# First MLP step taken row by row: centring, rounding and the order of TensorE's first products

## The reference

```python
# 1. retention: q, k, v (2, 8, 768, 64), blocks of 64 with decay lam per head -> x (2, 768, 512)
# 2. mixing:
X = np.fft.fft(x, axis=1)            # along the sequence
X = np.fft.fft(X, axis=2)            # along the features
u = x + np.real(X)
mu = np.mean(u, axis=-1, keepdims=True)
var = np.mean((u - mu) ** 2, axis=-1, keepdims=True)
un = (u - mu) / np.sqrt(var + 1e-06)
x = u + np.maximum(un @ w_ch1, 0.0) @ w_ch2          # w_ch1 (512, 2048), w_ch2 (2048, 512)
# 3. gate: five-tap causal convolution over the sequence, sigmoid, times (x @ w_val), times w_out
```

## Time and profile before

| | |
|---|---|
| time, median of 3 runs | 427.54 us (427.39 to 428.16) |
| the profiled execution's own time | 427.97 us |
| its span in the trace | 426.3 us |
| TensorE busy | 418.8 us, 98% of the span |
| VectorE, ScalarE, GpSimd busy | 281.3, 187.0 and 211.4 us |
| granted TensorE clock, mean | 1.00 |

### The profile page before, as it was taken

The page is one execution under the profiler, slowest core; times in us unless marked ns, Lnnn a source line. Parts: engine busy times, 40 slices in busy tenths (PEclk is TensorE's granted clock), DMA queues, the critical chain, the costliest instruction groups (busy, mean ns, idle before and its releaser), DMA issues.

```text
span 426.3 us, 6828 instructions
## 1 busy us (share of the span) xinstructions
PE 418.8 (98%) x2626; PEld 353.6 (83%) x2626; DVE 281.3 (66%) x451; ACT 187.0 (44%) x354; POOL 211.4 (50%) x139
## 2 busy tenths in 40 slices
PE   8999999999999999989999999999999999999997
PEld 8788888788888888879898988888788888888886
DVE  5658989759345579948667652617998859669400
ACT  2355842584213457474644432254254342624212
POOL 3543431443876396857787793445645338300000
PEclk9999999999999999999999999999999999999999
DMA  7997801430420231232232323321321321002022
GB/s 235 352 330 228 255 3 33 144 120 8 143 98 24 78 100 49 92 106 99 100 100 98 101 98 110 119 81 64 121 68 37 100 93 49 0 2 99 0 100 98
DMA packets 14863, 44.09 MB, mean 103 GB/s; under 512 B 1904, under 2 KB 2160, under 8 KB 14832
## 3 DMA queue, kind: packets, MB, share of 16 engines
q1 hardware_dynamic: 14832, 43.67, 30.9%
HBM read 40.52 MB, written 3.15 MB: 102 GB/s over the span
## 4 chain that ended last, share of the span: by engine, by line
PE 81%; DVE 12%; ACT 2%; DMA 2%; issue 2%; SPq 1%; DVEq 0%; ACTq 0%
PE ps L732 8%; PE ps L734 8%; PE ps L733 8%; PE ps L661 6%; PE ps L669 6%; PE ps L662 6%; PE ps L568 3%; PE ps L840 3%; PE ps L839 3%; PE ps L838 3%; PE ps L816 3%; PE ps L530 3%; PE ps L817 3%; PE ps L818 3%; PE ps L676 3%; PE ps L675 3%
## 5 line engine op out<-in xcount | busy, mean ns | idle before, releaser
L984 ACT ACTIVATE hh<-ps 128x512 fp32r<-128x512 f32 x32 | 18.9, 603 | 88.3 <-PE ps L669 88.3
L1358 DVE SCALAR_TENSOR_TENSOR hl<-ps,hh 128x512 fp32r<-128x512 f32 x32 | 21.6, 688 | 49.2 <-ACT hh L984 49.2
L1442 DVE SCALAR_TENSOR_TENSOR xT<-u_pad,cw,xT 128x768 f32<-128x768 f32 (+2 forms) x48 | 52.6, 1164 | 0.0
L1595 POOL TENSOR_TENSOR w2l_b<-raw_b,w2h_b 128x1024 fp32r<-128x1024 f32 x12 | 30.7, 2557 | 32.3 <-ACT w2h_b L947 32.3
L1595 POOL TENSOR_TENSOR w2l_a<-raw_a,w2h_a 128x1024 fp32r<-128x1024 f32 x12 | 31.1, 2592 | 29.9 <-ACT w2h_a L947 26.4
L732 PE MATMUL ps<-hh,w2h_a 128*128 128x512 f32 x96 | 37.9, 395 | 1.6 <-DVE xT L1374 1.6
L732 PE MATMUL ps<-hh,w2h_b 128*128 128x512 f32 x96 | 38.1, 397 | 0.1
L734 PE MATMUL ps<-hh,w2l_b 128*128 128x512 f32 x96 | 37.9, 395 | 0.0
L733 PE MATMUL ps<-hl,w2h_b 128*128 128x512 f32 x96 | 37.9, 395 | 0.0
L734 PE MATMUL ps<-hh,w2l_a 128*128 128x512 f32 x96 | 37.5, 391 | 0.0
L733 PE MATMUL ps<-hl,w2h_a 128*128 128x512 f32 x96 | 37.5, 390 | 0.0
(11 more groups left out here) (252 smaller groups left out, 1193.0 us busy)
## 6 DMA issues: line engine op xcount, KB each, us to landing
raw_a<-in_mlp SPq DMA_DIRECT2D x25, 512.0 KB, 3.6
raw_b<-in_mlp SPq DMA_DIRECT2D x23, 512.0 KB, 3.6
chunks<-in_qkv SPq DMA_DIRECT2D x12, 512.0 KB, 6.4
chunks<-in_qkv SPq DMA_DIRECT2D x22, 256.0 KB, 5.7
out<-out_sb SPq DMA_DIRECT2D x11, 256.0 KB, 2.0
raw_a<-in_val SPq DMA_DIRECT2D x2, 512.0 KB, 3.7
raw_b<-in_out SPq DMA_DIRECT2D x2, 512.0 KB, 5.5
seq_c<-const_seq SPq DMA_DIRECT2D x1, 768.0 KB, 7.9
```

The costliest lines, as they stand in the source:

```text
L984: nc.scalar.activation(hh[:, slot, j], ps[j][:, :], ACT.Relu).then_inc(s_hh, 1)
L1358: stt(hl[:, slot, j], ps[j][:, :], 0.0, hh[:, slot, j].bitcast(F32), ALU.max, ALU.subtract).then_inc(s_hl, 1)
L1442: stt(xT[:, b, r, tok], u_pad[b][:, r, PAD - d + tok.start:PAD - d + tok.stop], cw[:, K - 1 - d, r:r + 1], xT[:, b, r, tok], ALU.mult, ALU ...
L1595: tt(lo, raw_, hi.bitcast(F32), ALU.subtract).then_inc(s_w2l, 1)
```

## The change

On ScalarE and VectorE the first piece goes row by row: `centre(0)` is four instructions of one row, each counting `s_cen`, and `cen_hi(0)` four copies, each waiting for its own row. The counts that others wait for follow (`centred(i)` is the count at which piece i is centred). VectorE's `centre(1)` stands ahead of `radix4(N - 1)` and of step 0's low part. On TensorE step 0 has a function of its own, `first_hidden()`: the products of the high parts of the tokens for both banks come first, then those of the low parts for both. Behind it, and ahead of step 1's first layer, stand now `hid_transform(N - 2)` and `hid_transform(N - 1)`, the transforms 10 and 11.

```diff
         def high_parts(i):
-            return 2 * (i + 1) - (i >= 2)
+            return centred(i) - (i >= 2)
+
+        def centred(i):
+            return R + 2 * i
...
-                if n == NC + 4:
-                    pe.wait_ge(s_cen, 4)
+                if n >= NC + 4:
+                    pe.wait_ge(s_cen, centred(n - NC - 4))
...
             def mlp_hidden(st):
-                if st.m == 0:
-                    pe.wait_ge(s_pr, 2 * N)
...
+            def first_hidden():
+                pe.wait_ge(s_pr, 2 * N)
+                pe.wait_ge(s_w1h, 1)
+                pe.wait_ge(s_w1l, 1)
+                for j in range(2):
+                    cols = slice(j * P, (j + 1) * P)
+                    for r in range(R):
+                        if j == 0:
+                            pe.wait_ge(s_cenh, r + 1)
+                        mm(ps[j][:, :], w1h_a[:, r, cols], cen_h0[:, r], start=r == 0, stop=False)
+                        mm(ps[j][:, :], w1l_a[:, r, cols], cen_h0[:, r], start=False, stop=False)
+                for j in range(2):
+                    cols = slice(j * P, (j + 1) * P)
+                    for r in range(R):
+                        if j == 0 and r % 2 == 0:
+                            pe.wait_ge((s_cenl[0], s_cenl[1])[r // 2], r // 2 + 1)
+                        m = mm(ps[j][:, :], w1h_a[:, r, cols], cen_l0[:, r], start=False, stop=r == R - 1)
+                    m.then_inc(s_h, 1)
...
-            mlp_hidden(steps[0])
+            first_hidden()
+            hid_transform(N - 2)
+            hid_transform(N - 1)
...
                 if after:
                     mlp_hidden(after)
-                if st.m == 0:
-                    hid_transform(N - 2)
-                    hid_transform(N - 1)
...
             def cen_hi(i):
+                if i == 0:
+                    for r in range(R):
+                        act.wait_ge(s_cen, r + 1)
+                        copy(of_block(cen_h, i)[:, r], of_batch(acc_of, i)[:, r]).then_inc(s_cenh, 1)
+                    return
...
                 mu = wide(i)
+                if i == 0:
+
+                    for r in range(R):
+                        tt(of_batch(acc_of, i)[:, r], of_batch(u, i)[:, r], mu, ALU.subtract).then_inc(s_cen, 1)
+                    return
...
             centre(0)
             cen_lo(0)
+            centre(1)
             radix4(N - 1)
             hidden_lo(steps[0])
-            centre(1)
```

More of the change, by code:

```diff
@@ L638, in variance @@
                 pe.wait_ge(s_vl, b + 1)
-                pe.wait_ge(s_cen, 2 * len(pieces))
+                pe.wait_ge(s_cen, centred(len(pieces) - 1))
                 if b:
@@ L950, in squares @@
                 b = pieces[i].b
-                act.wait_ge(s_cen, 2 * (i + 1))
+                act.wait_ge(s_cen, centred(i))
                 act.wait_ge(s_mean, 2 * (b + 1))
@@ L971, in cen_hi @@
                     pair = slice(2 * e, 2 * e + 2)
-                    act.wait_ge(s_cen, 2 * i + e + 1)
+                    act.wait_ge(s_cen, centred(i) + e - 1)
                     if i == 2 and e == 0:
@@ L1277, in cen_lo @@
             def cen_lo(i):
-                dve.wait_ge(s_cenh, high_parts(i) - 1)
+                dve.wait_ge(s_cenh, high_parts(i) - 1 if i else 2)
                 tt(of_block(cen_l, i)[:, 0:2], of_batch(acc_of, i)[:, 0:2], of_block(cen_h, i)[:, 0:2].bitcast(F32),
@@ L1282, in cen_lo @@
                 if i == 0:
-                    dve.wait_ge(s_cenh, 2)
+                    dve.wait_ge(s_cenh, R)
                     tt(of_block(cen_l, i)[:, 2:4], of_batch(acc_of, i)[:, 2:4], of_block(cen_h, i)[:, 2:4].bitcast(F32),
@@ L1291, in combine_tokens @@
                 (b11, b21), (b12, b22) = ([of_batch(acc_of, i)[:, 2 * d:2 * d + 2] for d in range(2)] for i in (1, 2))
-                dve.wait_ge(s_cen, 6)
+                dve.wait_ge(s_cen, centred(2))
                 dve.wait_ge(s_f, 4 * R)
```

## The result

| | before | after |
|---|---|---|
| median, 6 runs each | 427.55 us (427.39 to 428.16) | 429.28 us (428.62 to 429.47) |
| profiled execution | 427.97 | 429.47 |
| its span | 426.3 | 427.7 |

The ratio of the times is 1.0034, 95% interval 1.0022 to 1.0047, or +1.45 us (0.94 to 2.0). It is estimated from all the runs; the two medians by themselves lie 1.73 us apart. Measured again beside the kernel before, with more runs, the ratio was 1.0021 (1.0009 to 1.0034), +0.9 us. The forecast was +0.92.

The account below looks back on a forecast made before the run. TensorE, busy 98% of the span, was taken to bound the kernel. A gain of 0.83 us from rows and a loss of 1.75 from the moved transforms gave +0.92, so 428.5 us, range 427.7 to 429.1 (8 in 10).

Parts of the forecast that it names:

- What bounds the kernel: Whole span: TensorE busy 98%; time won or lost between step 0's first layer and the MLP's middle goes on.
- Rows one by one: Start of step 0's first layer: row-wise centring and rounding gain 0.83 us, bounds 0.56 and 1.22.
- High parts first: Step 0's product order: changes nothing; low parts ready by 79.6, wanted at about 80.1, otherwise a microsecond late.
- the gain of the rows "alone": Start of step 0, forecast for the kernel with the transforms back: about 0.75 us gained, ratio 0.998.
- The moved transforms: Transform 10 behind step 0: TensorE waits 1.51 us for spectrum copies plus 0.24 restart, loss 1.75 us.
- The sum: Whole kernel: -0.83 + 1.75 = +0.92 us, giving 428.5 us, slower by 0.21%.
- The wait on the copies: Rival at transform 10: copies are ready, wait does not bind, only the gain stays, 426.7 us; chance 0.05.
- second late wait: Rival in the second batch, at 107.57 or from 147 to 191: 0.5 to 1.5 us more; chance 0.08.
- The clock: Rival after the new 1.5 us wait: TensorE's clock falls, 2.3 us for 10 products, 430.8 us; chance 0.02.

Follow-up runs that it names:

- old order: Kernel with the copies first, but step 0's products per bank, high parts then low parts; first mean to step 1's second layer 28.30 us, ratio 1.0001.
- transforms back: Changed kernel with transforms 10 and 11 back behind step 1's first layer; first mean to step 1's second layer 28.38 us, ratio 0.9999.
- only the transforms moved: Kernel before with only transforms 10 and 11 moved behind step 0's first layer and centre(1) ahead of chunk 11's fold; ratio 1.0035.
- copies first: Changed kernel with ScalarE's spectrum copies of transforms 8 and 9 ahead of step 0's two relus; 427.13 us, ratio 0.9970.
- the change again: Changed kernel without edit, timed again beside the kernel before; ratio 1.0021, first mean to step 1's second layer 29.30 us.
- Copies first, pairs: Kernel with the copies first, but piece 0 centred and rounded in pairs of rows as before; ratio 0.9999.

## Why the prediction was right, step by step

**What bounds the kernel.** Held. From step 1's second layer to the end the traces of before and of the change take 324.32 and 324.22 us, and the eight others lie between these, so what happened at 77 to 92 us went unchanged to the end. The wait near 191 moved along (191.48 to 192.95) and stayed 1.6, as I had read from VectorE's idle time at 146.69.

**Rows one by one.** Forecast 0.83, measured 0.75 or 0.76. The chain of waits of the changed kernel, to be held against the earlier trace rows:

```profile
76.93 0.25 PE ps L684
...
79.15 0.23 PE ps L684
...
80.99 1.85 PE ps L691 x8
...
84.32 0.71 PE ps L592 x4
...
92.68 0.23 PE ps L754
```

Transform 9 ends at 76.93 instead of 76.42, so 0.51 us are to be taken off each time of this trace. The four rows then started at 76.20, 76.74, 77.31 and 77.90; I had 76.26, 76.72, 77.30 and 77.89. Step 0 ended at 80.99 + 1.85 - 0.51 = 82.33, I had 82.26. Most of the 0.07 between these lies behind the rows: the last 16 products took 3.69 us (79.15 to 82.84), and I had 3.64. VectorE's four rows took 2.48 us, that is 0.60 apart at 0.68 each; I had 0.59. The prediction also gave a rule of the Trainium skill ("VectorE: DVE Perf Modes", "The DRAIN you can't avoid") by which each row would start only after the one before it had emptied the pipe, 0.68 apart, 2.72 for the four. I had read that section too narrowly: it says as well that a next operation that is not held starts earlier. The trace agrees with that sentence, and not with the rule taken alone.

**High parts first, at nothing.** The reason that I gave held (the low parts would have come late, and did in "old order"), and its price in the change is nothing. The size was off: I had the second pair a microsecond late, because I took it to be wanted together with the first, at 78.5; it is wanted two products later, and in "old order" it started 0.58 late. Nor were the low parts wanted at 78.5 in the kernel before, as I wrote, but at 79.25. And I named only half of what the order does. It frees bank 0 late, and I did not say what covers that: the moved transforms. That this term came out right is luck, since the cover happened to be part of the change; the gain of the rows "alone" that I put on record for the kernel with the transforms back was wrong for this reason, by 0.8 us.

**The moved transforms.** Forecast a loss of 1.75; measured 1.75 by itself ("only the transforms moved") and 1.80 in the change (29.32 against 27.52 with the copies first). In the change TensorE's wait ended at 83.81, with the 0.51 taken off, and I had 83.77. The first four products afterwards took 0.71 us in the chain instead of 0.44, 0.27 more for the restart where I had put 0.24.

**The sum.** +0.92 forecast, +1.00 and +0.98 measured in the stretch (in the chain, 92.68 - 0.51 against 91.16: 1.01). The time moved by 1.45 in the first comparison and by 0.9 in the second. In the traces of before and of the change what goes beyond the 1.00 is the 0.50 at the start, and "the change again" showed that the start varies by itself. That the same is behind the 1.45 of all runs is likely and not shown. My range reached to +1.6 for the spread of medians, and the spread was needed: +1.45 lies within it, but not within the +1.3 that the terms gave, and the median itself, 429.28, stands 0.2 above the 429.1 that I had named as the upper end. The size of the change's own effect in the traces needed none of it.

**The rivals.** The wait on the copies did bind. No second late wait came: VectorE ended the second batch's fold 5.1 us before TensorE wanted it, where I had counted on 4.8 and part of it lost:

```profile
103.27 0.69 DVE L1251 SCALAR_TENSOR_TENSOR yy<-sd,yy 128x514 f32<-128x514 f32 x1
...
109.07 0.38 PE L616 MATMUL ps<-seq_c,yy 128*128 128x128 f32 x2
```

The clock did not fall behind the new wait; the windows of the change (length, busy time of TensorE, its weight loads, VectorE, ScalarE and GpSimd, granted clock, DMA share, GB/s) show 1.00, the 2.4 GHz level, in it and behind it:

```profile
82.00:84.30 2.30, 0.82 (x4) 0.35 (x2) 1.63 (x4) 1.98 (x9) 1.97 (x1) 1.00 0.00 0
84.30:88.00 3.70, 3.68 (x21) 3.29 (x22) 0.00 (x0) 3.70 (x8) 0.53 (x2) 1.00 0.46 146
```

## What to carry to other kernels

Work that is moved to fill a gap takes its waits along. Look up what the thing waited for is queued behind on its own engine: here five copies stood behind a relu that needed the very last product, so the filling could not start until the gap was over, and moving one line behind two others on ScalarE turned +1.0 us into -0.8. Second, an edit that brings a result forward pays only if the next thing wanted is also early and the buffer it leaves is free in time; try the parts in pairs before calling one of them useless. Third, compare stretches between two fixed instructions in the traces. The one here repeated within 0.02 us in the two traces of the same kernel, where the first mean alone scattered by 0.9 over the ten traces.

## What was not expected of the hardware

The start of an execution varies more than all the rest. The first mean, at about 73.7 us, stood anywhere between 73.39 and 74.26 in ten traces, while what follows step 1's second layer took 324.22 to 324.32 in all ten. A late start of chunk 0's first product (5.19 to 5.77) did not go with a late mean in every trace: 5.48 went with 73.39, and 5.29 with 74.26. These two show where the scatter lies. "Transforms back", chunk 3's first product and the first mean:

```profile
17.31 1.16 PE L534 MATMUL ps<-chunks 64*128 64x128 f32 x16 [0.43 <-DMA chunks<-in_qkv]
...
74.26 1.45 PE L636 MATMUL ps<-out_sb,ones 128*128 128x512 f32 x4
```

"Copies first, pairs":

```profile
16.45 1.16 PE L534 MATMUL ps<-chunks 64*128 64x128 f32 x16
...
73.39 1.45 PE L636 MATMUL ps<-out_sb,ones 128*128 128x512 f32 x4
```

From chunk 3's first product to the first mean both take 56.95 or 56.94 us, and all ten traces lie between 56.94 and 56.96. So the whole scatter arises in the first 17 us. There TensorE waits in every trace at least once for a load of `in_qkv`, for 0.2 to 1.1 us at a time and at a different chunk from trace to trace. That these waits make up the scatter is likely; they were not added up.
